# The inverse of the attention's sums moved from VectorE's reciprocal to ScalarE's logarithm and exponential, and the turning of the maxima moved behind key tile 3

## The chip, the cores and the metric

The kernel runs on one core of one Trainium2 chip. The metric is the device time of one execution in microseconds. Three runs of the kernel before took 669.23, 670.58 and 672.26 us; the median is 670.58 us. PE is TensorE, ACT is ScalarE, DVE is VectorE, POOL is GpSimd, SP is SyncE, whose queue issues most DMAs.

## The reference, cut to what matters

Three stages follow each other: attention in which a query sees only the keys of its own hash bucket, a dense layer with a softmax gate and a layer norm (called SoLU here), and a mixture of eight experts with one expert for each token. The change touches only the attention:

```python
mask = q_bucket[:, :, :, None] == k_bucket[:, :, None, :]
scores = scale * np.matmul(q, k.transpose(0, 1, 3, 2))      # 16 heads, 768 x 768, depth 64
scores = np.where(mask, scores, -1000000000.0)
scores = scores - np.max(scores, axis=-1, keepdims=True)
attn = np.exp(scores)
attn = attn / (np.sum(attn, axis=-1, keepdims=True) + 1e-09)
return np.matmul(attn, v).astype(np.float32)
```

The kernel doesn't divide the weights. It multiplies weights by values first, and then scales the 64 x 768 result of a head by the inverse of each query's sum.

## The kernel before, in words

The attention takes the 16 heads one after the other (`for h in range(HEADS)`), each in six key tiles kt of 128 keys. Each engine has its own instruction list, written out by hand in program order, and the lists meet at semaphores. There is no scheduler: an instruction that waits holds everything behind it on its engine.

Head h on each engine:

- PE, for each kt: first two matmuls of a head further on, which produce scores only for finding maxima (`leading`, L472, head h+2 from kt 2 on, absent in heads 14 and 15), then four matmuls for the two query halves (`products`, L492 and L493). After the products of kt 2 come the sums of head h-1 (`sums(h-1)`, L514, which need all five adds of POOL for that head), the second half of its values (`values`, L504), and then `turn_maxima(h+1)` (L479), a transposition that writes bank RB of PSUM, the bank that also holds the sums. After kt 5 comes the first half of head h's values, which waits until DVE has finished head h-1 (`s_fin`). Heads 0, 2, 4, 6, 8 and 10 end with `hashes` for a later pair of heads.
- ACT: exponentials of the scores for each kt in two halves (`weights_of`, L1033); between them `weights_scaled(h)` (L1046) and, right behind kt 2, `weights_high(h)` (L1050), which prepare one piece of the next stage's weights. In odd heads up to 11 two copies of a later pair (`high_parts`, L1042) stand behind kt 0.
- POOL: in odd heads up to 11 `low_parts` (L1237), then `add(h, 1)` (L1248), then `weights_low(h)` (L1253), which waits for `weights_high(h)` of ACT, then the adds of kt 2 to 5 (L1248). Together the five adds form the head's sums over key tiles.
- DVE: maxima of `leading` (`maximum`, L728); for head h-1 `sums_out` (L748, which adds EPS and takes the sums out of PSUM), three reciprocals of 128 columns each (`inverse`, L753) with `maximum(h+2, 1)` between the second and the third, and `attended` (L759 and L763, which scales the head's result and raises `s_fin`); then `place_maxima(h+1)` (L741).

The semaphores that matter below: `s_acc` (adds of POOL done), `s_wh` (high part of a weight piece done), `s_rb` (sums in bank RB), `s_rec` (steps of DVE on the inverse), `s_fin` (head finished), `s_mt` (maxima turned).

Of the kernel before, what the change touches and what calls it, by code (L numbers as in the profile page):

```python
# [39 lines left out]
ACT = mybir.ActivationFunctionType  # L40
# [3 lines left out]
P = 128  # L44
B, H, S, D = 2, 8, 768, 64
NBITS = 6
HEADS = B * H
TILES = S // P
KT = S // P
HALF = S // 2  # L50
# [4 lines left out]
E = 8  # L55
# [11 lines left out]
EPS = 1e-9  # L67
# [21 lines left out]
C_SLOT = C_LOW + E * E  # L89
C_TOK = C_SLOT + SLOTS  # L90
C_ALT = C_TOK + NT
C_ALL = C_ALT + E - 1


def constants():

    c = np.zeros((P, C_ALL), np.float32)
    c[:, C_ID:C_ID + P] = np.eye(P)


    for group in range(4):
        for head in range(2):
            for n, sign in enumerate((1, -1) if group % 2 == 0 else (-1, 1)):
                r = slice(group * GROUP + head * BITS + n * NBITS, group * GROUP + head * BITS + (n + 1) * NBITS)
                c[r, C_THR] = LEAST if sign > 0 else -ABOVE
                c[r, C_TOP] = -BIG if group % 2 == 0 else 1.0
                if group < 2:
                    c[:, C_SIGN:C_SIGN + P][:, r] = sign
    c[:, C_TRI:C_TRI + P] = np.triu(np.ones((P, P)), 1)
    c[:, C_ONE:C_ONE + P] = 1  # L110
    c[:, C_EXP:C_EXP + E] = np.arange(E) - E
    c[:, C_J:C_J + NT] = np.arange(NT) * P


    c[:, C_J] = -1
    c[:, C_LOW:C_LOW + E * E] = np.tril(np.ones((E, E)), -1).reshape(1, -1)
    c[:, C_SLOT:C_SLOT + SLOTS] = np.arange(SLOTS)
    for n in range(NT):
        c[:, C_TOK + n] = (n % B) * S + (n // B) * P + np.arange(P)
    c[:, C_ALT:C_ALT + E - 1] = (-1.0) ** np.arange(E - 1)  # L120
    return c


# [11 lines left out]
def build(nc, qT, kT, vP, proj_d, w_solu, g_ln, w_gates, w1, w2, cst_d, out):  # L135
    with ExitStack() as ctx:
# [8 lines left out]
        cst = sb("cst", [P, C_ALL])  # L145
# [43 lines left out]
        def many(name, word, n, width, dt=F32):  # L189
            return [at(f"{name}{i}", word + i * width, [P, width], dt)[:, :] for i in range(n)], word + n * width  # L190
# [5 lines left out]
        xch, w = many("xch", 0, 2, DM, F32R)  # L196
        xcl, w = many("xcl", w, 2, DM, F32R)
# [8 lines left out]
        A1, w = many("A1", mid, SETS, S, F32R)  # L206
# [11 lines left out]
        PT = PT.rearrange("p (k g q) -> p k g q", k=KT, g=2)  # L218
        w = (w + 7) // 8 * 8
        acc, w = many("acc", w, 2, S)  # L220
        (rec,), w = many("rec", w, 1, HALF)
        stg, w = many("stg", w, 2, DM)
        empty = at("empty", mid - 2 * DM, [P, ROW])

# [37 lines left out]
        ld_w = [sem(f"ld_w{c}") for c in range(2)]  # L262
        s_high, s_low, s_ws, s_wh, s_wl = sem("s_high"), sem("s_low"), sem("s_ws"), sem("s_wh"), sem("s_wl")
        ld_v = [sem(f"ld_v{c}") for c in range(2)]
        (s_hash, s_bits, s_slot, s_nm, s_mm, s_mt, s_mc, s_st, s_exp, s_acc, s_pv, s_rb, s_rec,
         s_fin, s_ones, s_zeros) = [sem(n) for n in ("s_hash", "s_bits", "s_slot", "s_nm", "s_mm", "s_mt", "s_mc",
                                            "s_st", "s_exp", "s_acc", "s_pv", "s_rb", "s_rec", "s_fin", "s_ones", "s_zeros")]


        m_xh = sem("m_xh")  # L270
# [24 lines left out]
        def wait(eng, s, v):  # L295

            if not isinstance(v, int) or v > 0:
                eng.wait_ge(s, v)
# [153 lines left out]
        def _(pe):  # L452
# [22 lines left out]

            def turn_maxima(h):
                pe.wait_ge(s_mm, h + 1)
                wait(pe, s_rec, 6 * (h - 1) - 5)
                m = pe.transpose(PS[0:TILES, RB, 0:P], mm_[:, h % 2 * TILES:(h % 2 + 1) * TILES], ident)  # L479
                m.then_inc(s_mt, 1)  # L480

# [59 lines left out]
            for h in range(HEADS):  # L541
                for kt in range(KT):
                    ahead = (h + 1, kt + TILES - 2) if kt < 2 else (h + 2, kt - 2)
                    if ahead[0] < HEADS:
                        leading(*ahead)
                    products(h, kt)
                    if kt == 2:
                        if h > 0:
                            sums(h - 1)
                            values(h - 1, (3, 4, 5))  # L550
                        if h + 1 < HEADS:
                            turn_maxima(h + 1)
                values(h, (0, 1, 2))
                if h % 2 == 0 and h // 2 + 2 < PAIRS:
                    pe.wait_ge(s_mc, h + 2)
                    hashes(h // 2 + 2, RB)
# [150 lines left out]
        def _(dve):  # L707
# [35 lines left out]
                                  ident[0:TILES, 0:TILES].unsqueeze(2).broadcast_to([TILES, TILES, P]),  # L743
                                  ALU.mult).then_inc(s_mc, 1)

            def sums_out(h):
                dve.wait_ge(s_rb, h + 1)
                dve.tensor_scalar(rec, PS[:, RB, 0:HALF], EPS, None, ALU.add).then_inc(s_rec, 1)  # L748

            def inverse(h, n):  # L750

                dve.wait_ge(s_rec, 6 * h + 1)
                dve.reciprocal(rec[:, n * P:(n + 1) * P], rec[:, n * P:(n + 1) * P]).then_inc(s_rec, 1)  # L753

            def attended(h):

                p, c = h // 2, h % 2
                dve.wait_ge(s_pv, 2 * h + 2)
                dve.tensor_copy(mu[:, c:c + 1], PS[:, PVB, HALF:HALF + 1]).then_inc(s_rec, 1)  # L759
                dve.wait_ge(s_rec, 6 * h + 5)  # L760
                for g in range(2):
                    mine = slice(g * D, (g + 1) * D)
                    m = dve.scalar_tensor_tensor(  # L763
                        out=xT[c * D:(c + 1) * D, p * S + g * HALF:p * S + (g + 1) * HALF], in0=PS[mine, PVB, 0:HALF],
                        scalar=mu[mine, c:c + 1], in1=rec[mine, :], op0=ALU.add, op1=ALU.mult)
                    m.then_inc(s_rec if g == 0 else s_fin, 1)
# [36 lines left out]
            for h in range(HEADS):  # L803
                if h + 1 < HEADS:
                    maximum(h + 1, TILES - 2)
                    maximum(h + 1, TILES - 1)
                    maxima(h + 1)
                if h % 2 == 1 and h // 2 + 2 < PAIRS:
                    hash_bits(h // 2 + 2, RB)
                if h + 2 < HEADS:  # L810
                    maximum(h + 2, 0)
                if h > 0:
                    sums_out(h - 1)
                    inverse(h - 1, 0)
                    inverse(h - 1, 1)
                if h + 2 < HEADS:
                    maximum(h + 2, 1)
                if h > 0:
                    inverse(h - 1, 2)
                    attended(h - 1)  # L820
                if h + 1 < HEADS:
                    place_maxima(h + 1)
                if h + 2 < HEADS:
                    maximum(h + 2, 2)
                    maximum(h + 2, 3)
            sums_out(HEADS - 1)
            for n in range(3):
                inverse(HEADS - 1, n)
            attended(HEADS - 1)
            soft(0, 0, True)  # L830

# [190 lines left out]
        def _(act):  # L1022
            fn = nc.scalar.activation

            act.dma_start(hashw[:, :], proj_d).then_inc(s_cst, 16)
            act.dma_start(cst[:, :], cst_d).then_inc(s_cst, 16)

            def weights_of(h, kt, g):
                act.wait_ge(s_st, 2 * (KT * h + kt) + g + 1)
                if h > 0 and g == 0:  # L1030
                    act.wait_ge(s_pv, 2 * h - 1 if kt < 3 else 2 * h)
                    act.wait_ge(s_acc, (KT - 1) * (h - 1) + max(kt, 1))
                fn(PT[:, kt, g, 0:HALF], PS[:, STB + g, 0:HALF], ACT.Exp, scale=SCALE).then_inc(s_exp, 1)  # L1033

            def high_parts(p):
                act.wait_ge(ld_r[p % 2], 32 * (p // 2) + 32)
                if p > 0:
                    for h in (2 * p - 2, 2 * p - 1):
                        ready_1(act, h)
                        ready_2(act, h)  # L1040
                for r, high in zip(R[p % 2], (Hq, Hk)):
                    fn(high, r, ACT.Copy).then_inc(s_high, 1)  # L1042

            def weights_scaled(m):
                act.wait_ge(ld_w[m % 2], 16 * (m // 2) + 16)
# [2 lines left out]
            def weights_high(m):  # L1048
                act.wait_ge(s_ws, m + 1)
                fn(piece(m, 0), stg[m % 2], ACT.Copy).then_inc(s_wh, 1)  # L1050
# [26 lines left out]
            for h in range(HEADS):  # L1077
                weights_of(h, 0, 0)
                weights_of(h, 0, 1)
                if h % 2 == 1 and h // 2 + 2 < PAIRS:  # L1080
                    high_parts(h // 2 + 2)
                weights_of(h, 1, 0)
                weights_of(h, 1, 1)
                weights_scaled(h)
                weights_of(h, 2, 0)
                weights_of(h, 2, 1)
                if h == HEADS - 1:
                    act.wait_ge(s_rows0, 16 * SLOTS)
                weights_high(h)
                for kt in (3, 4, 5):  # L1090
                    weights_of(h, kt, 0)
                    weights_of(h, kt, 1)
                if h == HEADS - 2:
                    act.wait_ge(s_fin, HEADS // 2)
                    take(0, 0, 0, True)
            soft(0, 0, True)
            act.wait_ge(s_fin, HEADS)
            take(1, 1, 0, True)
# [263 lines left out]
```

## Time and profile before

| what | value |
|---|---|
| median of three runs | 670.58 us |
| the profiled execution | 669.12 us, span 667.0 us |
| mean granted TensorE clock | 0.956 |
| PE busy | 584.1 us (88%) |
| DVE busy | 402.7 us (60%) |
| POOL busy | 268.8 us (40%) |
| ACT busy | 258.7 us (39%) |
| chain that ended last | PE 75%, ACT 5%, issue 5%, DVE 4%, DMA 4%, POOL 3% |
| three reciprocals a head (L753) | 48 instructions, 42.9 us, 927 ns each |

The span is the time from the first to the last instruction in the profile; the execution's own time is 2.1 us longer. The busy shares are averages over three stages. The attention lies in roughly the first 246 us of the span, the SoLU layer ends near 400 us, and the experts take the rest. The change touches the first of these.

### The profile page before, as it was taken

What the parts mean: (1) busy time and instruction counts of PE and PEld (TensorE: products, weight loads), DVE (VectorE), ACT (ScalarE), POOL (GpSimd) and SP (SyncE); (2) the same over time, 40 slices, a digit from 0 to 9 for tenths busy, and PEclk for the clock granted to TensorE, in tenths of its full rate; (3) what the DMA queues carried; (4) which work ended last, traced back from release to release, by engine and by line L of the source; (5) the groups of instructions that cost most, each with busy time, mean ns of one, the idle gap of its engine ahead of it and who ended that gap; (6) DMA issues with size and microseconds to landing.
All of it is one profiled execution on the core that took longest, in us unless ns stands there. A gap on an engine that the chain in (4) does not pass through costs nothing.

```text
span 667.0 us, 9761 instructions
## 1 busy us (share of the span) xinstructions
PE 584.1 (88%) x2886; PEld 437.3 (66%) x2887; DVE 402.7 (60%) x557; ACT 258.7 (39%) x403; POOL 268.8 (40%) x188
## 2 busy tenths in 40 slices
PE   3889999999999979999999996108999999999994
PEld 1566556556566447888888874007887878788773
DVE  3659888888899546556656662724266455556511
ACT  1255454546554522222222243124255364464410
POOL 4378879888887832322332235530000000100101
PEclk9999999999999998999999997558999999999997
DMA  6789578696571011000000003277146645755400
GB/s 188 168 227 242 155 212 213 158 261 171 124 199 29 12 59 68 1 1 0 0 0 0 0 1 126 91 258 259 56 167 209 240 159 179 270 163 180 151 4 30
DMA packets 39266, 83.90 MB, mean 126 GB/s; under 512 B 7485, under 2 KB 10429, under 8 KB 39232
## 3 DMA queue, kind: packets, MB, share of 16 engines
q1 hardware_dynamic: 31376, 71.04, 36.0%
q10 hardware_dynamic: 5616, 6.12, 3.6%
q0 software_dynamic: 2240, 6.31, 2.4%
q8 instruction: 18, 0.29, 0.2%
q14 instruction: 16, 0.13, 0.1%
HBM read 52.09 MB, written 12.35 MB: 97 GB/s over the span
## 4 chain that ended last, share of the span: by engine, by line
PE 75%; ACT 5%; issue 5%; DVE 4%; DMA 4%; POOL 3%; SPq 2%; ACTq 2%; DVEq 0%; POOLq 0%
PE PS L504 9%; PE PS L492 5%; PE PS L662 5%; PE PS L664 4%; PE PS L663 4%; PE PS L472 4%; PE PS L493 4%; PE PS L535 4%; PE PS L643 3%; PE PS L537 3%; PE PS L536 3%; PE PS L644 3%; PE PS L645 3%; PE PS L576 3%; PE PS L578 3%
## 5 line engine op out<-in xcount | busy, mean ns | idle before, releaser
L1033 ACT ACTIVATE at_PT<-PS 128x384 f32<-128x384 f32 x192 | 84.5, 491 | 100.5 <-PE PS L493 99.8
L1248 POOL TENSOR_TENSOR at_acc<-at_acc,at_PT 128x768 f32<-128x768 f32 x64 | 108.0, 1687 | 8.7 <-ACT at_PT L1033 2.8
L958 DVE TENSOR_TENSOR at_W<-at_raw,at_W 128x2048 f32 (+1 forms) x30 | 67.8, 2289 | 70.8 <-ACT at_W L1103 68.2
L728 DVE TENSOR_REDUCE sb_nm<-PS 128x1 f32<-128x768 f32 x96 | 90.2, 955 | 23.1 <-PE PS L472 18.5
L1324 POOL DMA_INDIRECT out<-at_yb,sb_to x16 | 15.8, 986 | 204.9 <-DVE at_yb L970 204.9
L1103 ACT ACTIVATE at_W<-at_raw 128x2048 f32 (+1 forms) x32 | 60.2, 1910 | 60.3 <-issue 34.5
L492 PE MATMUL PS<-at_A,at_B 102*128 102x384 f32 x192 | 75.1, 391 | 7.6 <-ACT at_PT L1033 7.6
L504 PE MATMUL PS<-at_PT,at_V 128*64 128x385 f32 x384 | 68.4, 489 | 2.4 <-ACT at_PT L1033 2.4
L493 PE MATMUL PS<-at_A,at_B 128*128 128x384 f32 x192 | 66.9, 349 | 0.0
L1279 POOL TENSOR_TENSOR at_cn<-at_eb,sb_mv 128x1024 f32<-128x1024 f32 x12 | 22.7, 1896 | 108.0 <-DVE sb_mv L784 108.0
L472 PE MATMUL PS<-at_B,at_A 76*128 76x384 f32 x192 | 57.9, 390 | 6.7 <-DMA at_B<-at_HB 4.7
L662 PE MATMUL PS<-at_W,at_hTh 128*128 x128 | 52.3, 408 | 5.9 <-DVE at_hTl L989 5.6
L492 PEld LDWEIGHTS PS<-at_A,at_B 102*128 102x128 f32 x192 | 37.5, 196 | 26.6 <-ACT at_PT L1033 20.4
L643 PE MATMUL PS<-at_W,at_xsh 128*128 x128 | 52.1, 407 | 3.2 <-DVE at_xsl L962 3.2
L664 PE MATMUL PS<-at_W,at_hTl 128*128 x128 | 50.5, 394 | 0.0
L644 PE MATMUL PS<-at_W,at_xsh 128*128 x128 | 50.5, 394 | 0.0
L645 PE MATMUL PS<-at_W,at_xsl 128*128 x128 | 50.4, 394 | 0.0
L663 PE MATMUL PS<-at_W,at_hTh 128*128 x128 | 50.4, 394 | 0.0
L504 PEld LDWEIGHTS PS<-at_PT,at_V 128*64 128x64 f32 x384 | 28.0, 136 | 34.2 <-issue 25.8
L472 PEld LDWEIGHTS PS<-at_B,at_A 76*128 76x128 f32 x192 | 36.3, 211 | 20.4 <-DVE sb_nm L728 13.2
L535 PE MATMUL PS<-at_wsp,at_xch 128*128 128x512 f32 x96 | 39.9, 415 | 4.6 <-POOL at_xcl L1258 4.6
L753 DVE RECIPROCAL at_rec<-at_rec 128x128 f32<-128x128 f32 x48 | 42.9, 927 | 0.6
(154 smaller groups left out, 1099.5 us busy)
## 6 DMA issues: line engine op xcount, KB each, us to landing
at_raw<-w SPq DMA_DIRECT2D x32, 1024.0 KB, 5.4
at_A<-at_H SPq DMA_DIRECT2D x32, 192.0 KB, 2.7
at_B<-at_H SPq DMA_DIRECT2D x28, 192.0 KB, 3.7
rows_by_expert<-at_empty SPq DMA_DIRECT2D x19, 257.0 KB, 5.3
at_XS<-rows_by_expert ACTq DMA_DIRECT2D x17, 256.0 KB, 2.7
at_stg<-w_solu SPq DMA_DIRECT2D x16, 256.0 KB, 4.1
at_V<-vP SPq DMA_DIRECT2D x16, 192.0 KB, 3.9
at_Re<-qT SPq DMA_DIRECT2D x4, 384.0 KB, 5.0
```

What stands on the lines that cost most here:

```text
L472: m = mm(slot(h, j)[:, g, :], A1[t][0:ROWS1, j * P:(j + 1) * P], B1[t][0:ROWS1, g * HALF:(g + 1) * HALF], start=True, stop=True)
L492: mm(PS[:, STB + g, 0:HALF], B1[t][0:ROWS, at_k], A1[t][0:ROWS, at_g], start=True, stop=False)
L493: mm(PS[:, STB + g, 0:HALF], B2[t][:, at_k], A2[t][:, at_g], start=False, stop=True).then_inc(s_st, 1)
L504: m = mm(PS[g * D:(g + 1) * D, PVB, 0:HALF + 1], V[h % 2][:, kt, :], PT[:, kt, g, :], start=(kt == 0), stop=(kt == KT - 1))
L643: mm(PS[:, g, :], xsh[:, x_k], W[:, high], start=(k == 0), stop=False)
L644: mm(PS[:, g, :], xsh[:, x_k], W[:, low], start=False, stop=False)
L662: mm(PS[:, 4 + c, :], hTh[:, h_f], W[:, high], start=(f == 0), stop=False)
L663: mm(PS[:, 4 + c, :], hTh[:, h_f], W[:, low], start=False, stop=False)
L664: m = mm(PS[:, 4 + c, :], hTl[:, h_f], W[:, high], start=False, stop=(f == FB - 1))
L728: dve.tensor_reduce(nm[:, col:col + 1], slot(h, j), AX.XY, ALU.max, negate=True).then_inc(s_nm, 1)
L1033: fn(PT[:, kt, g, 0:HALF], PS[:, STB + g, 0:HALF], ACT.Exp, scale=SCALE).then_inc(s_exp, 1)
L1248: pool.tensor_tensor(total, PT[:, 0, :, 0:HALF] if kt == 1 else total, PT[:, kt, :, 0:HALF], ALU.add).then_inc(s_acc, 1)
```

## The change

The inverse of a head's sums is computed in another way. ACT takes the logarithm of the sum plus EPS straight out of PSUM into `rec`, and then exp(-x) of it in place. DVE makes one Newton step: the first instruction forms err = (sum + EPS) * rec, the second rec = (2 - err) * rec. The two replace `sums_out` and the three reciprocals. `maximum(h+2, 1)` now stands ahead of both.

On ACT the two new instructions stand behind the exponentials of kt 2, and `weights_high(h)` moves from there to behind those of kt 3. On PE `turn_maxima(h+1)` moves from behind the values of kt 2's block to behind the products of kt 3, and its wait on `s_rec` now names the first Newton instruction of head h-1, which is the last reader of bank RB. An activation table set that holds both functions is loaded by name at the start. The constants grow by one column with EPS in it, and a buffer `err` of 384 columns joins `rec`.

```diff
-        (rec,), w = many("rec", w, 1, HALF)
+        (rec, err), w = many("rec", w, 2, HALF)
...
             def turn_maxima(h):
                 pe.wait_ge(s_mm, h + 1)
-                wait(pe, s_rec, 6 * (h - 1) - 5)
+                wait(pe, s_rec, 4 * (h - 1) - 3)
...
                             values(h - 1, (3, 4, 5))
-                        if h + 1 < HEADS:
-                            turn_maxima(h + 1)
+                    if kt == 3 and h + 1 < HEADS:
+                        turn_maxima(h + 1)
...
-            def sums_out(h):
-                dve.wait_ge(s_rb, h + 1)
-                dve.tensor_scalar(rec, PS[:, RB, 0:HALF], EPS, None, ALU.add).then_inc(s_rec, 1)
-
-            def inverse(h, n):
-
-                dve.wait_ge(s_rec, 6 * h + 1)
-                dve.reciprocal(rec[:, n * P:(n + 1) * P], rec[:, n * P:(n + 1) * P]).then_inc(s_rec, 1)
+            def inverse(h):
+
+                dve.wait_ge(s_ln, 2 * h + 2)
+                dve.scalar_tensor_tensor(out=err, in0=PS[:, RB, 0:HALF], scalar=EPS, in1=rec,
+                                         op0=ALU.add, op1=ALU.mult).then_inc(s_rec, 1)
+                dve.wait_ge(s_rec, 4 * h + 1)
+                dve.scalar_tensor_tensor(out=rec, in0=err, scalar=2.0, in1=rec, reverse0=True,
+                                         op0=ALU.subtract, op1=ALU.mult).then_inc(s_rec, 1)
...
                 if h + 2 < HEADS:
                     maximum(h + 2, 0)
-                if h > 0:
-                    sums_out(h - 1)
-                    inverse(h - 1, 0)
-                    inverse(h - 1, 1)
                 if h + 2 < HEADS:
                     maximum(h + 2, 1)
                 if h > 0:
-                    inverse(h - 1, 2)
+                    inverse(h - 1)
                     attended(h - 1)
...
+            act.preload_act_table_set("natural_log_exp_and_others")
...
+            def inverse(h):
+
+                act.wait_ge(s_rb, h + 1)
+                wait(act, s_fin, h)
+                fn(rec, PS[:, RB, 0:HALF], ACT.Ln, bias=cst[:, C_EPS:C_EPS + 1]).then_inc(s_ln, 1)
+                act.wait_ge(s_ln, 2 * h + 1)
+                fn(rec, rec, ACT.Exp, scale=-1.0).then_inc(s_ln, 1)
...
                 weights_of(h, 2, 0)
                 weights_of(h, 2, 1)
+                if h > 0:
+                    inverse(h - 1)
                 if h == HEADS - 1:
                     act.wait_ge(s_rows0, 16 * SLOTS)
-                weights_high(h)
                 for kt in (3, 4, 5):
                     weights_of(h, kt, 0)
                     weights_of(h, kt, 1)
+                    if kt == 3:
+                        weights_high(h)
```

ACT in head 2, before, from the scaling of the weight piece on. at_stg is the piece, at_wsp its high part, at_PT the exponentials of one half, those of kt 2 in the second and third row.

```order
L1046 ACTIVATE at_stg_85<-at_stg_85,sb_gcol 128x512 [waits ld_w0]
L1033 ACTIVATE at_PT_81<-PS 128x384 [waits s_acc,s_pv,s_st]
L1033 ACTIVATE at_PT_81<-PS 128x384 [waits s_st]
L1050 ACTIVATE at_wsp<-at_stg_85 128x512 [waits s_ws]
L1033 ACTIVATE at_PT_81<-PS 128x384 [waits s_acc,s_pv,s_st]
L1033 ACTIVATE at_PT_81<-PS 128x384 [waits s_st]
```

The same place now. L1045 is the logarithm, L1047 the exponential of its negative, L1055 the high part of the piece.

```order
L1051 ACTIVATE at_stg_86<-at_stg_86,sb_gcol 128x512 [waits ld_w0]
L1030 ACTIVATE at_PT_81<-PS 128x384 [waits s_acc,s_pv,s_st]
L1030 ACTIVATE at_PT_81<-PS 128x384 [waits s_st]
L1045 ACTIVATE at_rec_84<-PS,sb_cst 128x384 [waits s_fin,s_rb]
L1047 ACTIVATE at_rec_84<-at_rec_84 128x384 [waits s_ln]
L1030 ACTIVATE at_PT_81<-PS 128x384 [waits s_acc,s_pv,s_st]
L1030 ACTIVATE at_PT_81<-PS 128x384 [waits s_st]
L1055 ACTIVATE at_wsp<-at_stg_86 128x512 [waits s_ws]
```

The high part has gone behind the two exponentials of kt 3, and two instructions on at_rec stand in its old place. POOL's list is unchanged: its wait on `s_wh` is still between the first and the second add.

PE in head 3, before, from the last values matmuls of head 2 on. sb_mm are the maxima being turned, at_B_64 and at_A_56 belong to the leading matmuls of head 5.

```order
L504 MATMUL PS<-at_PT_81,at_V_79 64x385 x5
L479 MATMUL PS<-sb_cst,sb_mm 6x128 [waits s_rec,s_mm]
L472 MATMUL PS<-at_B_64,at_A_56 128x384 [waits s_nm]
L472 MATMUL PS<-at_B_64,at_A_56 128x384
L492 MATMUL PS<-at_A_58,at_B_66 128x384 [waits s_exp]
L493 MATMUL PS<-at_A_62,at_B_70 128x384
L492 MATMUL PS<-at_A_58,at_B_66 128x384 [waits s_exp]
L493 MATMUL PS<-at_A_62,at_B_70 128x384
L472 MATMUL PS<-at_B_64,at_A_56 128x384 [waits s_nm]
```

The same place now (L481 is the turning).

```order
L506 MATMUL PS<-at_PT_81,at_V_79 64x385 x5
L474 MATMUL PS<-at_B_64,at_A_56 128x384 [waits s_nm]
L474 MATMUL PS<-at_B_64,at_A_56 128x384
L494 MATMUL PS<-at_A_58,at_B_66 128x384 [waits s_exp]
L495 MATMUL PS<-at_A_62,at_B_70 128x384
L494 MATMUL PS<-at_A_58,at_B_66 128x384 [waits s_exp]
L495 MATMUL PS<-at_A_62,at_B_70 128x384
L481 MATMUL PS<-sb_cst,sb_mm 6x128 [waits s_rec,s_mm]
L474 MATMUL PS<-at_B_64,at_A_56 128x384 [waits s_nm]
```

The turning has passed the leading matmuls and products of kt 3 and stands, with its two waits, ahead of the leading matmuls of kt 4.

## Rows read from the trace of the kernel before

**Rows 1.** Windows: stretch, its us, busy us by engine, TensorE clock, DMA share, GB/s.
```profile
20.00:60.00 40.00, 35.03 (x153) 25.01 (x155) 27.37 (x36) 19.20 (x39) 27.38 (x17) 1.00 0.80 204
...
100.00:140.00 40.00, 38.60 (x210) 23.89 (x211) 34.12 (x47) 20.96 (x47) 35.05 (x23) 1.00 0.79 197
250.00:255.00 5.00, 3.98 (x9) 3.15 (x10) 3.84 (x10) 0.00 (x0) 3.79 (x3) 0.50 0.59 239
```

**Rows 2.** Timeline of PE, the sums: start, us, engine, line, operation, count, [idle before].
```profile
112.83 0.87 PE L514 MATMUL PS<-at_acc,sb_cst 128*64 128x384 f32 x4
...
127.11 0.87 PE L514 MATMUL PS<-at_acc,sb_cst 128*64 128x384 f32 x4
...
139.57 0.87 PE L514 MATMUL PS<-at_acc,sb_cst 128*64 128x384 f32 x4
...
217.99 0.87 PE L514 MATMUL PS<-at_acc,sb_cst 128*64 128x384 f32 x4
...
229.50 0.87 PE L514 MATMUL PS<-at_acc,sb_cst 128*64 128x384 f32 x4
...
240.65 0.87 PE L514 MATMUL PS<-at_acc,sb_cst 128*64 128x384 f32 x4
```

**Rows 3.** Timeline of PE inside head 6, around the maxima and the values.
```profile
112.56 0.33 PE L493 MATMUL PS<-at_A,at_B 128*128 128x384 f32 x1
...
115.57 0.27 PE L479 MATMUL PS<-sb_cst,sb_mm 128*6 128x128 f32 x1
115.59 0.60 PE L472 MATMUL PS<-at_B,at_A 76*128 76x384 f32 x2
...
116.74 0.51 PE L472 MATMUL PS<-at_B,at_A 76*128 76x384 f32 x2
...
119.00 0.34 PE L493 MATMUL PS<-at_A,at_B 128*128 128x384 f32 x1
119.52 2.16 PE L504 MATMUL PS<-at_PT,at_V 128*64 128x385 f32 x12 [0.18 <-ACT at_PT L1033]
```

**Rows 4.** Timeline of ACT in head 6, and one row of head 14.
```profile
112.74 0.86 ACT L1033 ACTIVATE at_PT<-PS 128x384 f32<-128x384 f32 x2
113.48 0.64 ACT L1050 ACTIVATE at_wsp<-at_stg 128x512 fp32r<-128x512 f32 x1
116.58 0.87 ACT L1033 ACTIVATE at_PT<-PS 128x384 f32<-128x384 f32 x2 [2.46 <-PE PS L493]
...
221.39 0.87 ACT L1033 ACTIVATE at_PT<-PS 128x384 f32<-128x384 f32 x2 [2.12 <-PE PS L493]
```

**Rows 5.** Timeline of POOL in heads 6 and 7.
```profile
114.20 1.29 POOL L1253 TENSOR_TENSOR at_wsp<-at_stg,at_wsp 128x512 fp32r<-128x512 f32 x1 [0.35 <-ACT at_wsp L1050]
...
130.22 1.31 POOL L1253 TENSOR_TENSOR at_wsp<-at_stg,at_wsp 128x512 fp32r<-128x512 f32 x1
131.46 7.19 POOL L1248 TENSOR_TENSOR at_acc<-at_acc,at_PT 128x768 f32<-128x768 f32 x4
```

**Rows 6.** Timeline of DVE in head 6, and at the end of the attention.
```profile
116.23 0.96 DVE L728 TENSOR_REDUCE sb_nm<-PS 128x1 f32<-128x768 f32 x1
117.11 0.94 DVE L753 RECIPROCAL at_rec<-at_rec 128x128 f32<-128x128 f32 x1
...
118.11 1.26 DVE L763 SCALAR_TENSOR_TENSOR at_xT<-PS,sb_mu,at_rec 64x384 f32<-64x384 f32 x2
...
246.43 1.23 DVE L772 TENSOR_REDUCE sb_nm<-PS 128x1 f32<-128x1024 f32 x1 [0.38 <-PE PS L537]
```

**Rows 7.** Timeline of all engines at the first tiles of the SoLU layer.
```profile
249.49 1.27 POOL L1258 TENSOR_TENSOR at_xcl<-at_xT,at_xch 128x512 fp32r<-128x512 f32 x1 [10.19 <-ACT at_xch L1063]
...
251.02 0.77 PE L535 MATMUL PS<-at_wsp,at_xch 128*128 128x512 f32 x1 [4.62 <-POOL at_xcl L1258]
...
251.98 1.90 POOL L1279 TENSOR_TENSOR at_cn<-at_eb,sb_mv 128x1024 f32<-128x1024 f32 x1 [1.22 <-DVE sb_mv L784]
...
252.13 1.76 DVE L789 TENSOR_TENSOR sb_var_all<-sb_var_all,sb_rs 128x1 f32<-128x1 f32 x1
```

More of the change, by code:

```diff
@@ L91 @@
 C_ALT = C_TOK + NT
-C_ALL = C_ALT + E - 1
+C_EPS = C_ALT + E - 1
+C_ALL = C_EPS + 1
 def constants():
@@ L120, in constants @@
     c[:, C_ALT:C_ALT + E - 1] = (-1.0) ** np.arange(E - 1)
+    c[:, C_EPS] = EPS
     return c
@@ L264, in build @@
         ld_v = [sem(f"ld_v{c}") for c in range(2)]
-        (s_hash, s_bits, s_slot, s_nm, s_mm, s_mt, s_mc, s_st, s_exp, s_acc, s_pv, s_rb, s_rec,
+        (s_hash, s_bits, s_slot, s_nm, s_mm, s_mt, s_mc, s_st, s_exp, s_acc, s_pv, s_rb, s_ln, s_rec,
          s_fin, s_ones, s_zeros) = [sem(n) for n in ("s_hash", "s_bits", "s_slot", "s_nm", "s_mm", "s_mt", "s_mc",
-                                            "s_st", "s_exp", "s_acc", "s_pv", "s_rb", "s_rec", "s_fin", "s_ones", "s_zeros")]
+                                            "s_st", "s_exp", "s_acc", "s_pv", "s_rb", "s_ln", "s_rec", "s_fin", "s_ones", "s_zeros")]
         m_xh = sem("m_xh")
@@ L759, in attended @@
                 dve.tensor_copy(mu[:, c:c + 1], PS[:, PVB, HALF:HALF + 1]).then_inc(s_rec, 1)
-                dve.wait_ge(s_rec, 6 * h + 5)
+                dve.wait_ge(s_rec, 4 * h + 3)
                 for g in range(2):
@@ L825, in _ @@
                     maximum(h + 2, 3)
-            sums_out(HEADS - 1)
-            for n in range(3):
-                inverse(HEADS - 1, n)
+            inverse(HEADS - 1)
             attended(HEADS - 1)
@@ L1095, in _ @@
                     take(0, 0, 0, True)
+            inverse(HEADS - 1)
             soft(0, 0, True)
```

## The prediction

> **What bounds the kernel now.** I read the windows by stage first, then the timelines of PE, ACT, POOL and DVE over one head, and then the waits between them. From 100 to 140 us PE is busy for 38.60 of 40 us at a clock of 1.00, DVE for 34.12, POOL for 35.05, ACT for 20.96 [rows 1]. So PE bounds the attention, and POOL is close behind; ACT has room.
>
> I measure a head by the start of its sums matmuls, S. Between S = 127.11 and 139.57 lie 12.46 us, between 112.83 and 127.11, where hashes and two copies of ACT stand too, 14.28 us; the last two intervals take 229.50 - 217.99 = 11.51 and 240.65 - 229.50 = 11.15 [rows 2]. By the loops there are 15 intervals: eight of the first kind, five of the second (hashes stand in heads 2, 4, 6, 8 and 10), and the last two, where the leading matmuls are gone.
>
> One wait of PE inside a head matters. The values of kt 0 to 2 start 0.52 us after the last product, at 119.00 and 119.52, where the same step ahead of the sums takes 0.27 (112.56 to 112.83) [rows 2, 3]. The profile names ACT with 0.18, but those exponentials were done long before. What ended was DVE's scaling of the previous head, at 118.11 + 1.26 = 119.37 [rows 6], and PE followed 0.15 later. So PE loses 0.25 a head to `s_fin`.
>
> **The change part by part.**
>
> *ACT's new work: nothing.* The sums end at S + 0.87 [rows 2]. ACT sits idle for 2.46 us before the exponentials of kt 3, which start at 116.58 = S + 3.75, and the copy that leaves gives 0.64 more [rows 4]. The two new instructions have 384 columns each; the nearest row is a pair of exponentials of that size in 0.87 us, so about 1.0 with their semaphore. They may take up to 2.8 before kt 3 is late, and DVE asks for them only at S + 4.26 (below). A slower logarithm would have to be three times an exponential to show.
>
> *The moved copy: on the path.* POOL's second instruction on the weight piece waits for it, and the four adds of kt 2 to 5 stand behind that in POOL's list. Without the turning the exponentials of kt 3 start 0.02 sooner (the turning shifts the next matmul by 115.59 - 115.57 [rows 3]), at S + 3.73. The second ACT slot behind a pair is at 113.48 - 112.74 = 0.74 [rows 4], so the copy runs from S + 4.47 to S + 5.11, and POOL starts 0.08 later (114.12 to 114.20 [rows 4, 5]), at S + 5.19. Today it does so at S + 1.37. The rest is fixed: 1.24 to the first add (130.22 to 131.46), 7.19 for four adds [rows 5], and 0.25 from POOL's end to PE (250.76 to 251.02 [rows 7]). The next S is therefore at S + 5.19 + 1.24 + 7.19 + 0.25 = S + 13.87 at the earliest. In odd heads POOL also has `low_parts` ahead of this, two instructions that end well before S + 5.
>
> *DVE's Newton step: reads PSUM late.* It stands behind `maximum(h+2, 1)`, which starts at 116.23 and lets the next instruction start at 117.11 [rows 6], that is S + 4.28, now 4.26. For each step I take 0.6, the nearest row being the scaling, two of 384 columns in 1.26 us; lower bound 0.49, one exponential of that size, upper bound the 0.94 of a reciprocal, of only 128 columns. The first step ends at S + 4.86, the second runs from 4.90 to 5.50.
>
> *The lock.* The second step reads two SBUF operands. At 252.13 a DVE operation on one column with two such operands takes 1.76 us and ends at 253.89; POOL's instruction that started at 251.98 ends at 253.88 [rows 7]. So such a DVE operation and a POOL operation do not run together, and the later one waits. Here DVE comes at S + 4.90 and POOL at S + 5.19: POOL waits until 5.50, and the interval becomes 5.50 + 1.24 + 7.19 + 0.25 = 14.18. The Trainium skill (SBUF — State Buffer, "Who interferes with whom") says that a VectorE instruction with two SBUF inputs contends with a GpSimd instruction that reads SBUF and that whichever issues first blocks the other. By that rule, the trace agrees; without it the interval would be the 13.87.
>
> *The turning behind kt 3: a new wait of PE.* It waits for the first Newton step of head h-1, the last reader of bank RB. PE is ready at 116.74 = S + 3.91 [rows 3], where the leading matmuls of kt 4 start today. The step ends at S + 4.86, with 0.15 to PE that is 5.01, and those matmuls start at 5.03: 1.12 later. Behind it on PE stand kt 4 and 5, the values, and the hashes. The 0.25 at `s_fin` goes: PE comes to the values at 6.43 + 1.12 = S + 7.55, DVE's scaling ends at about 5.58 + 1.26 = 6.84, so PE is last. Net 1.12 - 0.25 = 0.87 where PE sets the interval.
>
> *What leaves.* Three reciprocals and the copy out of PSUM leave DVE, which nothing waits for any longer. At the end of the attention DVE's chain is shorter, but its next reduction at 246.43 was released by PE [rows 6], so nothing is gained.
>
> **The sum.** In the eight plain intervals both waits stand side by side. PE alone would need 12.46 + 0.87 = 13.33, POOL's loop 14.18, so the loop decides: 8 x 1.72 = 13.8. In the five with hashes PE needs 14.28 + 0.87 = 15.15, more than the loop: 5 x 0.87 = 4.35. In heads 14 and 15 the sums go first to DVE, early enough for the turning and for the lock, and the kt 3 exponentials start at 221.39 = S + 3.40 [rows 2, 4], so the loop is 3.40 + 0.74 + 0.64 + 0.08 + 1.24 + 7.19 + 0.25 = 13.54, against 11.51 and 11.15: 2.03 + 2.39 = 4.4. In all 22.5 us. The profiled execution took 669.12, so 691.6; on the median of 670.58, which is 1.5 higher, 693.1.
>
> **The rivals.**
>
> *POOL wins the lock.* The margin is only 0.29 us. If POOL's low part starts first at 5.19, DVE waits until 5.19 + 1.27 = 6.46, the second step ends at 7.06, the adds start there, and the interval is 7.06 + 7.19 + 0.25 = 14.50: 8 x 0.32 = 2.6 more. The scaling would end at 7.06 + 0.15 + 1.26 = 8.47, PE go on at 8.62 instead of 7.55, 5 x 1.07 = 5.3 more where PE decides. That is 701. A Newton step longer than I take, or a DVE that is late by 0.3, does it.
>
> *The adds don't gate.* If POOL is faster on the four adds than in the row, or the sums are hidden by PE's own new wait, only the turning costs: 13 x 0.87 = 11.3, so 682. Against it: four adds took 7.19 in the row I use, and the gap to close is 0.85 us.
>
> *The relief of DVE counts: faster.* Place: `s_fin`. Were the new inverse ready so soon that `attended` ends before PE wants the values, PE would gain up to 0.25 in each of 13 heads, 3.3 us, and come to 667. It decides only if the maximum ahead of the inverse ends before S + 3.9 - 0.8, and if the loop over the weight piece stays under 12.46. Both fail by more than 1 us in the rows.
>
> *The clock falls.* PE would be busy for about 85% of a plain interval. From 20 to 60 us it was busy for 35.03 of 40 and the clock stayed at 1.00; after an idle stretch of 4.62 us it was 0.50 [rows 1, 7]. The new waits are at most 2.4 us. If they did it in only four heads, 12 us of PE work at half speed each would add some 48, so 740.
>
> *The change doesn't do what it says.* If the logarithm and exponential each brought a table load, ACT would need more than the gap it has. The instruction list has no such load in the attention, so I give this nothing of its own.
>
> **How the numbers follow.** Forecast 0.60, POOL first 0.18, adds not gating 0.11, clock 0.04, faster 0.03, something that cancels both waits 0.04. The predicted time is 693. The forecast's own range is 688 to 697, from steps of 0.49 to 0.94 us and the interval of 13.87. For 8 in 10 it must reach over the first rival and to the second: 682 to 701. About 0.5% (3.4 us) is what can be told from no change. Faster than that 0.03, within it 0.04, slower 0.93.
>
> **What would show it.** In the profile after, the sums of neighbouring plain heads should stand 14.2 us apart, with PE idle before the sums and released by POOL's adds, and the pairs with hashes 15.1 apart with no such wait. PE should sit idle for about 1.1 us before the turning, released by the first Newton step. POOL should wait before the weight piece until S + 5.2 or 5.5, and its four adds should take 7.2. ACT should still be idle before kt 3, and no table load should stand in the attention. The two later stages should have their old length. I'm wrong if POOL's low part still starts soon after the kt 2 exponentials, if the turning meets no wait, or if a second DVE step of nearly 2 us shows that POOL got the lock.

## The result, and the profile after

The changed kernel takes 690.9 us (median of four runs, 689.62 to 692.69). The ratio to the kernel before is 1.0307 with a 95% interval of 1.0273 to 1.0341: it is slower, by 20 us. The forecast was 693. The profiled execution took 692.69 us with a span of 690.9. It is the longest of the four, at a mean granted clock of 0.937, where the other three have 0.952 to 0.955; two of them lie at 689.6 and 689.7.

The first reading is the chain that ended last, on the page of the changed kernel, in shares of the span by engine. Before, PE held 75% of it and POOL 3%.

```profile
PE 48%; POOL 23%; issue 12%; ACT 4%; DVE 4%; DMA 4%; ACTq 2%; SPq 2%; DVEq 0%; POOLq 0%
```

POOL now holds 23%. The table of waits of the changed kernel, from 60 to 240 us, says who waited for whom: us in total, times, the longest.

```profile
POOL at_wsp L1262 <- ACT at_wsp L1055: 37.2, 13, 3.8
...
PE PS L481 <- DVE at_rec L751: 10.8, 12, 0.9
...
PE PS L516 <- POOL at_acc L1257: 3.7, 8, 0.5
```

Three waits that were not there, or nearly so: POOL for ACT's copy of the weight piece, PE at the turning (L481) for the first Newton step (L751), and PE at the sums (L516) for POOL's adds. The columns of the timelines below are those of [rows 2]: start, duration, engine, line, operation, count, and idle time before with its releaser. First PE, in head 6 of the changed kernel, which answers to [rows 2, 3].

```profile
120.39 0.33 PE L495 MATMUL PS<-at_A,at_B 128*128 128x384 f32 x1
121.19 0.87 PE L516 MATMUL PS<-at_acc,sb_cst 128*64 128x384 f32 x4 [0.47 <-POOL at_acc L1257]
...
123.92 0.62 PE L474 MATMUL PS<-at_B,at_A 76*128 76x384 f32 x2
...
124.91 0.33 PE L495 MATMUL PS<-at_A,at_B 128*128 128x384 f32 x1
126.15 0.27 PE L481 MATMUL PS<-sb_cst,sb_mm 128*6 128x128 f32 x1 [0.90 <-DVE at_rec L751]
126.17 0.59 PE L474 MATMUL PS<-at_B,at_A 76*128 76x384 f32 x2
...
128.63 2.16 PE L506 MATMUL PS<-at_PT,at_V 128*64 128x385 f32 x12
...
136.22 0.87 PE L516 MATMUL PS<-at_acc,sb_cst 128*64 128x384 f32 x4
```

The sums at 121.19 were held 0.47 us by POOL. The turning at 126.15 was held 0.90 us by DVE, where PE was ready at 125.25. The values at 128.63 carry no wait any more. From 121.19 to 136.22 lie 15.03 us, before 14.28. ACT in the same head, to be held against [rows 4]:

```profile
120.57 0.86 ACT L1030 ACTIVATE at_PT<-PS 128x384 f32<-128x384 f32 x2
122.10 0.58 ACT L1045 ACTIVATE at_rec<-PS,sb_cst 128x384 f32<-128x384 f32 x1 [0.67 <-PE PS L516]
122.71 0.52 ACT L1047 ACTIVATE at_rec<-at_rec 128x384 f32<-128x384 f32 x1
124.94 0.87 ACT L1030 ACTIVATE at_PT<-PS 128x384 f32<-128x384 f32 x2 [1.70 <-PE PS L495]
125.70 0.63 ACT L1055 ACTIVATE at_wsp<-at_stg 128x512 fp32r<-128x512 f32 x1
```

The logarithm takes 0.58 and the exponential 0.52, and 1.70 us of idle time is left ahead of kt 3. The copy (L1055) now starts at 125.70. POOL, against [rows 5]:

```profile
117.62 3.52 POOL L1257 TENSOR_TENSOR at_acc<-at_acc,at_PT 128x768 f32<-128x768 f32 x2
121.09 1.54 POOL L1257 TENSOR_TENSOR at_acc<-at_PT 128x768 f32<-128x768 f32 x1
126.40 1.36 POOL L1262 TENSOR_TENSOR at_wsp<-at_stg,at_wsp 128x512 fp32r<-128x512 f32 x1 [3.77 <-ACT at_wsp L1055]
127.73 7.18 POOL L1257 TENSOR_TENSOR at_acc<-at_acc,at_PT 128x768 f32<-128x768 f32 x4
```

POOL's instruction on the weight piece (L1262) waits until 126.40 = S + 5.21. The adds that PE waits for ended at 117.62 + 3.52 = 121.14, 0.05 ahead of the sums. DVE, against [rows 6]:

```profile
119.67 1.48 DVE L737 SCALAR_TENSOR_TENSOR sb_mm<-sb_nm 128x6 f32<-128x6 f32 x1
121.08 0.94 DVE L730 TENSOR_REDUCE sb_nm<-PS 128x1 f32<-128x768 f32 x1
124.58 0.96 DVE L730 TENSOR_REDUCE sb_nm<-PS 128x1 f32<-128x768 f32 x1 [2.56 <-PE PS L474]
125.45 0.55 DVE L751 SCALAR_TENSOR_TENSOR at_rec<-PS,at_rec 128x384 f32<-128x384 f32 x1
126.03 0.56 DVE L754 SCALAR_TENSOR_TENSOR at_rec<-at_rec,at_rec 128x384 f32<-128x384 f32 x1
126.51 0.15 DVE L761 COPY sb_mu<-PS 128x1 f32<-128x1 f32 x1
126.70 1.27 DVE L765 SCALAR_TENSOR_TENSOR at_xT<-PS,sb_mu,at_rec 64x384 f32<-64x384 f32 x2
```

The first step ends at 126.00 = S + 4.81. Nothing waits for the scaling (126.70). At 119.67 the turning's maxima, an instruction on six columns that took 0.17 in every head before, take 1.48 and end at 121.15, with POOL's add.

All intervals between the sums of neighbouring heads, worked out from the starts of the sums in the timelines (medians, where a column holds several; S is the start of a head's sums):

| kernel | S of head 0 | 0 to 1 | seven plain ones | five with hashes | 13 to 14 | 14 to 15 | S of head 15 |
|---|---|---|---|---|---|---|---|
| before | 46.90 | 12.46 | 12.46 | 14.28 | 11.51 | 11.15 | 240.65 |
| after | 48.52 | 15.08 | 13.76 | 15.03 | 13.32 | 15.08 | 263.47 |
| e1_copy_only | 47.40 | 16.01 | 13.69 | 14.35 | 13.32 | 13.38 | 257.77 |
| e2_copy_back | 48.10 | 14.95 | 13.75 (two of 14.1) | 15.91 | 11.67 | 11.25 | 262.44 |
| e3_inverse_first | 46.92 | 15.25 | 13.69 | 14.35 (one of 16.06) | 13.33 | 14.97 | 259.79 |
| e4_both | 47.74 | 13.79 | 12.21 (two of 12.87) | 14.68 (one of 15.14) | 11.67 | 11.28 | 245.13 |
| e5_step_after_max | 47.66 | 13.65 | 12.23 | 14.01 | 11.63 | 11.31 | 239.95 |
| e6_no_second_step | 47.66 | 14.83 | 13.23 | 15.04 | 11.50 | 11.12 | 252.90 |
| e7_err_in_psum | 48.33 | 13.27 | 12.21 | 14.01 | 11.49 | 11.11 | 239.75 |

For the changed kernel this makes 7 x 1.30 = 9.1 us in plain intervals, 5 x 0.75 = 3.8 with hashes, 2.6 in the first, 1.8 and 3.9 in the last two, and 1.6 before the first sums: 22.8 of the span's 23.9. The other 1.1 us lies behind the attention.

The first interval and the last are longer than their pattern by 1.3 and 1.7 us, and there the clock was lower (from 40 to 60 us a mean granted clock of 0.83, before 1.00). In head 1 of the changed kernel ACT waited 3.50 us for a DMA that fills at_B (0.69 before), PE sat idle for 4.48 us until ACT's exponentials were done (1.68 before), and behind that the four sums matmuls took 1.55 us instead of 0.87 and the twelve values matmuls 2.79 instead of 2.11. PE around the last interval, and two windows of the changed kernel (the columns of [rows 1]):

```profile
248.39 0.87 PE L516 MATMUL PS<-at_acc,sb_cst 128*64 128x384 f32 x4 [1.68 <-POOL at_acc L1257]
249.09 3.80 PE L506 MATMUL PS<-at_PT,at_V 128*64 128x385 f32 x12
```

```profile
245.00:250.00 5.00, 3.12 (x15) 1.51 (x16) 0.00 (x0) 2.91 (x7) 4.86 (x4) 0.92 0.00 0
250.00:255.00 5.00, 4.72 (x18) 1.97 (x14) 2.51 (x5) 1.91 (x5) 1.07 (x2) 0.74 0.00 0
```

The same twelve values matmuls take 2.11 us elsewhere and 3.80 here, after 1.68 us of waiting for POOL; the granted clock of the stretch from 250 to 255 is 0.74, a mixture of its two levels, 1.2 and 2.4 GHz.

### The profile page after: what moved, and what is told of

Its sections match the earlier page's. It is cut to its first block, busy times and chain, and to the rows that moved or that the text cites. A ratio compares the mean times of both kernels' runs of the same rounds, so it can differ in the third digit from the quotient of the medians.

```text
span 690.9 us, 9776 instructions
## 1 busy us (share of the span) xinstructions
PE 587.2 (85%) x2886; PEld 435.0 (63%) x2887; DVE 383.2 (55%) x525; ACT 276.2 (40%) x435; POOL 269.1 (39%) x188
## 4 chain that ended last, share of the span: by engine, by line
PE 48%; POOL 23%; issue 12%; ACT 4%; DVE 4%; DMA 4%; ACTq 2%; SPq 2%; DVEq 0%; POOLq 0%
POOL at_acc L1257 16%; PE PS L664 4%; PE PS L666 4%; PE PS L665 4%; PE PS L645 3%; PE PS L537 3%; PE PS L646 3%; PE PS L647 3%; PE PS L539 3%; PE PS L578 3%; PE PS L538 3%; PE PS L580 3%; PE PS L579 3%; POOL at_wsp L1262 3%; POOL rows_by_expert L1323 2%
## 5 line engine op out<-in xcount | busy, mean ns | idle before, releaser
L494 PE MATMUL PS<-at_A,at_B 102*128 102x384 f32 x192 | 73.1, 381 | 10.4 <-ACT at_PT L1030 10.3
L506 PE MATMUL PS<-at_PT,at_V 128*64 128x385 f32 x384 | 70.7, 504 | 0.0
L1288 POOL TENSOR_TENSOR at_cn<-at_eb,sb_mv 128x1024 f32<-128x1024 f32 x12 | 22.8, 1896 | 108.5 <-DVE sb_mv L786 108.5
L474 PEld LDWEIGHTS PS<-at_B,at_A 76*128 76x128 f32 x192 | 34.3, 205 | 28.2 <-issue 16.4
L578 PE MATMUL PS<-at_wsp,at_lnh 128*128 128x512 f32 x96 | 39.2, 408 | 1.7 <-DVE at_lnl L838 1.7
```

The costliest lines, as they stand in the source:

```text
L474: m = mm(slot(h, j)[:, g, :], A1[t][0:ROWS1, j * P:(j + 1) * P], B1[t][0:ROWS1, g * HALF:(g + 1) * HALF], start=True, stop=True)
L494: mm(PS[:, STB + g, 0:HALF], B1[t][0:ROWS, at_k], A1[t][0:ROWS, at_g], start=True, stop=False)
L506: m = mm(PS[g * D:(g + 1) * D, PVB, 0:HALF + 1], V[h % 2][:, kt, :], PT[:, kt, g, :], start=(kt == 0), stop=(kt == KT - 1))
```

## The experiments

The first four share the kernel before at 670.04 us (13 runs); the last three share 670.92 us (18 runs).

**e1_copy_only.** The kernel before, only the copy moved:

```diff
-                weights_high(h)
                 for kt in (3, 4, 5):
                     weights_of(h, kt, 0)
                     weights_of(h, kt, 1)
+                    if kt == 3:
+                        weights_high(h)
```

> The kernel before with one edit: ScalarE's copy weights_high(h) moved behind the exponentials of kt 3; reciprocals and turning as before. Theory (the loop over the weight piece): plain intervals between sums go from 12.46 to about 13.69 us (the 13.76 measured with the change, less the 0.07 that the lock cost), intervals with hashes stay at 14.28, the last two at 13.3 and 13.3 or more: 8 x 1.23 + 1.8 + 2.2 = 13.8 us slower, 684 to 687. Rival (the turning is what costs, the adds don't gate): intervals unchanged, 671.

Measured: 685.77 us, ratio 1.0230 (1.0192 to 1.0269). POOL in head 6, and PE at the sums ahead of and behind it:

```profile
124.73 1.29 POOL L1254 TENSOR_TENSOR at_wsp<-at_stg,at_wsp 128x512 fp32r<-128x512 f32 x1 [3.78 <-ACT at_wsp L1050]
125.98 7.17 POOL L1249 TENSOR_TENSOR at_acc<-at_acc,at_PT 128x768 f32<-128x768 f32 x4
```

```profile
119.51 0.87 PE L514 MATMUL PS<-at_acc,sb_cst 128*64 128x384 f32 x4 [1.17 <-POOL at_acc L1249]
...
133.86 0.87 PE L514 MATMUL PS<-at_acc,sb_cst 128*64 128x384 f32 x4
```

POOL starts on the piece at 124.73 = S + 5.22 and has its adds done at 133.15. The plain intervals are 13.69, as expected. The intervals with hashes became 14.35, where I expected 14.28. The adds are not the reason, since they end 0.71 ahead of the sums at 133.86, and PE's last product starts as late after S as before (14.00 against 14.01). What ends last is on DVE:

```profile
131.77 1.40 DVE L735 SCALAR_TENSOR_TENSOR sb_mm<-sb_nm 128x6 f32<-128x6 f32 x1
133.09 0.67 DVE L722 TENSOR_SCALAR at_HB<-PS,sb_cst 128x384 fp32r<-128x384 f32 x1
```

In these intervals the sums also wait for the hash bits of a later pair (L722, `s_bits`). The maxima's instruction ahead of them (L735) reads SBUF twice, now stands beside POOL's adds and takes 1.40 us, where it took 0.17 in every head before. So the bits end at 133.76, and the sums follow 0.10 later. This is read from the trace; no run takes it apart. So the moved copy alone, with reciprocals and turning as they were, makes 15.7 of the 20 us.

**e2_copy_back.** The changed kernel with the copy back at its old place:

```diff
+                weights_high(h)
                 if h > 0:
                     inverse(h - 1)
...
-                    if kt == 3:
-                        weights_high(h)
```

> The changed kernel with one edit: weights_high(h) back behind the exponentials of kt 2, ahead of the logarithm; turning behind kt 3 and Newton step stay. Theory A (only the wait of the turning is left, lock without effect): plain intervals 12.46 + 0.77 = 13.2, with hashes 15.03, last two as before: 13 x 0.76 = 10 us slower than before, 681. Theory B (the lock counts here): POOL now adds kt 3 from about S + 4.7 to 6.4 when the second Newton instruction wants to start at S + 4.8, so it waits up to 1.6 us and shows a duration near 2.1, the scaling ends at S + 8.3 and PE waits for it: 13 intervals 1.7 longer, 693, no better than the change. Theory C (loop irrelevant): 691 with intervals of 13.76.

Measured: 690.18 us, ratio 1.0290 (1.0254 to 1.0326). No better than the change, though POOL doesn't wait for the copy any more. DVE, POOL and PE in head 6:

```profile
127.18 1.96 DVE L754 SCALAR_TENSOR_TENSOR at_rec<-at_rec,at_rec 128x384 f32<-128x384 f32 x1
```

```profile
127.03 1.69 POOL L1256 TENSOR_TENSOR at_acc<-at_acc,at_PT 128x768 f32<-128x768 f32 x1 [0.39 <-ACT at_PT L1030]
```

```profile
127.29 0.27 PE L481 MATMUL PS<-sb_cst,sb_mm 128*6 128x128 f32 x1 [0.90 <-DVE at_rec L751]
...
130.66 2.16 PE L506 MATMUL PS<-at_PT,at_V 128*64 128x385 f32 x12 [0.81 <-DVE at_xT L765]
```

The second Newton step takes 1.96 us instead of 0.56. It asks at 127.18, while POOL's add of 127.03 to 128.72 runs; the next DVE instruction starts at 129.06. PE then waits 0.81 at the values for the scaling, on top of 0.90 at the turning. Theory B holds, with 690 where it said 693; over all 16 instructions the second step has a median of 1.86 us.

**e3_inverse_first.** The changed kernel with DVE's inverse ahead of the maximum:

```diff
-                if h + 2 < HEADS:
-                    maximum(h + 2, 1)
                 if h > 0:
                     inverse(h - 1)
+                if h + 2 < HEADS:
+                    maximum(h + 2, 1)
+                if h > 0:
                     attended(h - 1)
```

> The changed kernel with one edit on VectorE: both Newton instructions ahead of maximum(h+2, 1), so that the turning's wait is over before PE comes to it; the copy stays behind kt 3. Theory: the wait of 0.90 us before the turning goes, plain intervals stay at 13.7 (the loop over the weight piece sets them), those with hashes return from 15.03 to 14.0 to 14.3: 5 x 0.75 to 1.0 = 4 to 5 us faster than the change, 685 to 687. Rival (the turning sets all intervals): all 13 shorter by 0.8 to 1.0, 679.

Measured: 688.74 us (686.02 to 690.02), ratio 1.0268 (1.0222 to 1.0313), 2.2 under the change, where 4 to 5 was expected. PE from head 5 to 6:

```profile
108.46 0.27 PE L481 MATMUL PS<-sb_cst,sb_mm 128*6 128x128 f32 x1
...
111.05 2.16 PE L506 MATMUL PS<-at_PT,at_V 128*64 128x385 f32 x12
...
118.25 1.48 PE L516 MATMUL PS<-at_acc,sb_cst 128*64 128x384 f32 x4 [1.34 <-POOL at_acc L1258]
```

The turning at 108.46 waits for nothing. The intervals did as the theory said: 13.69 in the plain ones, 14.35 with hashes, as in e1_copy_only. With the turning's wait gone those with hashes could have been as short as the 14.01 of the last experiments. Again the sums follow the hash bits by 0.10: in the next head the maxima's instruction takes 1.60 us, the bits end at 134.21, the sums start at 134.31. One interval of 16.06 and the last of 14.97 took back 1.7 and 1.6 us. The times of this kernel and of the changed one overlap, so it is the intervals that tell them apart, and not the medians. In the row at 118.25 the sums take 1.48 us instead of 0.87, right behind an idle time of 1.34.

**e4_both.** Both edits together, e2_copy_back and e3_inverse_first.

> The changed kernel with both edits: weights_high(h) back behind kt 2 and both Newton instructions ahead of maximum(h+2, 1). Theory without lock: both waits gone, and VectorE's scaling done earlier, 13 x 0.25 less than before: 667 to 668. Theory with lock: the second Newton instruction starts at about S + 3.0 while POOL adds kt 2 (S + 2.6 to 4.3), waits there for 1.3 us in even heads, and pushes maximum(h+2, 1) and the scaling back: PE waits about 0.5 us more than before at the leading matmuls of kt 5 or the values, 674 to 678.

Measured: 670.97 us, ratio 1.0004 (0.9977 to 1.0031). All that the change cost is gone. The time fits neither theory as stated, 667 to 668 without the lock and 674 to 678 with it: the lock is there, but costs less than I had put on it. Intervals with hashes are 14.68 and those of heads 12 and 13 are 12.87. DVE, POOL and PE in an even head:

```profile
117.65 0.56 DVE L751 SCALAR_TENSOR_TENSOR at_rec<-PS,at_rec 128x384 f32<-128x384 f32 x1 [1.80 <-ACT at_rec L1048]
118.24 1.78 DVE L754 SCALAR_TENSOR_TENSOR at_rec<-at_rec,at_rec 128x384 f32<-128x384 f32 x1
119.94 0.94 DVE L730 TENSOR_REDUCE sb_nm<-PS 128x1 f32<-128x768 f32 x1
```

```profile
117.92 1.69 POOL L1257 TENSOR_TENSOR at_acc<-at_acc,at_PT 128x768 f32<-128x768 f32 x1
```

```profile
120.94 0.61 PE L474 MATMUL PS<-at_B,at_A 76*128 76x384 f32 x2 [0.34 <-DVE sb_nm L730]
```

The second step starts at 118.24, beside POOL's add of 117.92 to 119.61, and takes 1.78. The maximum behind it starts at 119.94, and PE's leading matmuls of kt 5 wait 0.34 for it. In plain intervals up to head 11 the step starts when POOL's add has only about 0.2 us left and takes 0.62 to 0.64, and it is POOL's instruction on the piece behind it that takes 1.61 to 1.64 instead of 1.29. They are 12.21, a quarter of a microsecond under the kernel before.

**e5_step_after_max.** e4_both, with the second Newton step (now in `refined`) behind the maximum:

```diff
                 if h > 0:
                     inverse(h - 1)
                 if h + 2 < HEADS:
                     maximum(h + 2, 1)
                 if h > 0:
+                    refined(h - 1)
                     attended(h - 1)
```

> The kernel of e4_both with one edit on VectorE: the second Newton instruction moved behind maximum(h+2, 1), the first stays ahead of it. The lock is still there, but the instruction now asks for it at about S + 4.25, when POOL's add of kt 2 (S + 2.6 to 4.3 in even heads) is ending and the next starts at S + 4.7. Theory (the lock made e4_both lose): the second instruction takes 0.55 to 0.7 instead of 1.78, intervals with hashes fall from 14.68 to 14.0, heads 12 and 13 from 12.87 to 12.2, plain ones stay at 12.2: 4 to 5 us under e4_both, 666 to 667. Rival (something else holds those heads): they stay at 14.68 and 12.87.

Measured: 668.21 us, ratio 0.9961 (0.9945 to 0.9977): faster than the kernel before, by 0.4%. DVE in head 8:

```profile
143.46 0.96 DVE L730 TENSOR_REDUCE sb_nm<-PS 128x1 f32<-128x768 f32 x1 [0.50 <-PE PS L474]
144.33 0.55 DVE L757 SCALAR_TENSOR_TENSOR at_rec<-at_rec,at_rec 128x384 f32<-128x384 f32 x1
```

The step takes 0.55 to 0.57 in 14 of 16 cases, the intervals are 12.23 and 14.01. In two, which lie in the last two intervals, it meets an add of POOL and takes 1.77. The kernel is 2.8 us under e4_both, where I expected 4 to 5. In the two profiled executions the sums of head 15 come 5.2 us sooner, a little more than expected, but from there to the end e4_both took 424.0 us and this kernel 426.2, as the kernel before did (426.4). So the difference to the expectation lies behind the attention; why it was shorter in e4_both isn't known.

**e6_no_second_step.** e2_copy_back without the second Newton step, a copy of one column in its place. The inverse is that of logarithm and exponential alone.

```diff
-                dve.scalar_tensor_tensor(out=rec, in0=err, scalar=2.0, in1=rec, reverse0=True,
-                                         op0=ALU.subtract, op1=ALU.mult).then_inc(s_rec, 1)
+                dve.tensor_copy(err[:, 0:1], err[:, 0:1]).then_inc(s_rec, 1)
```

> The kernel of e2_copy_back without the second Newton instruction: a copy of one column in its place, so the inverse is that of logarithm and exponential alone. The copy has one SBUF input. Theory (the second instruction waited for POOL's add in e2_copy_back, 1.62 to 1.96 us, and PE for it 0.81 us at the values): that wait goes, only the turning's 0.90 stays, plain intervals 13.2, with hashes 15.0: 10 us over before, 680 to 681. Rival (the hold came from elsewhere): intervals stay at 13.75 and 15.9, 690.

Measured: 679.73 us, ratio 1.0137 (1.0111 to 1.0163), 10.5 under e2_copy_back. PE in an even head:

```profile
124.00 0.27 PE L481 MATMUL PS<-sb_cst,sb_mm 128*6 128x128 f32 x1 [0.90 <-DVE at_rec L751]
...
126.49 2.16 PE L506 MATMUL PS<-at_PT,at_V 128*64 128x385 f32 x12
```

The wait of 0.90 at the turning is there, the one at the values is not; the intervals are 13.23 and 15.04. This kernel has the turning's wait by itself, and it costs 0.76 to 0.77 in each of the twelve intervals between heads 1 and 13.

**e7_err_in_psum.** e4_both, with the first step's result in PSUM, over the sums, instead of in SBUF:

```diff
-        (rec, err), w = many("rec", w, 2, HALF)
+        (rec,), w = many("rec", w, 1, HALF)
...
+        err = PS[:, RB, 0:HALF]
...
-                wait(pe, s_rec, 4 * (h - 1) - 3)
+                wait(pe, s_rec, 4 * (h - 1) - 2)
```

> The kernel of e4_both with one edit: the first Newton instruction writes its result over the sums in PSUM bank RB instead of into an SBUF buffer, so that the second has one SBUF and one PSUM input; the turning now waits for the second, which ends at about S + 3.6, before PE comes to it at S + 3.9. Same arithmetic, same order. Theory (two SBUF inputs are what locks): no instruction of 1.78 us any more, intervals 12.2, 14.0 and 12.2, 666 to 667, and POOL's low part falls back from 1.61 to 1.29. Rival (POOL and VectorE disturb each other whatever the operands): as e4_both, 671 with intervals of 14.68 and 12.87.

Measured: 667.88 us, ratio 0.9948 (0.9928 to 0.9968), the lowest median here, though not to be told from e5_step_after_max. The second step's 16 instructions (shortest, median, longest in ns, first and last start), and POOL in head 7:

```profile
L755 DVE SCALAR_TENSOR_TENSOR at_rec<-PS,at_rec x16: 557/557/558, 51.7 to 242.4; 128x384 f32<-128x384 f32 x16
```

```profile
131.17 1.30 POOL L1263 TENSOR_TENSOR at_wsp<-at_stg,at_wsp 128x512 fp32r<-128x512 f32 x1
132.43 7.20 POOL L1258 TENSOR_TENSOR at_acc<-at_acc,at_PT 128x768 f32<-128x768 f32 x4
```

With one operand in PSUM the same arithmetic at the same place (S + 2.95, in e4_both S + 2.94) takes 0.56 in all 16 cases, 15 of which lie beside an instruction of POOL; in e4_both the median was 1.77. POOL's instruction on the piece takes 1.30, where it took 1.61 in the same head there. The intervals are 12.21 and 14.01. So it is the two SBUF operands that lock here, and not that DVE and POOL work side by side. The Trainium skill (SBUF — State Buffer, "Who interferes with whom") states this for two SBUF inputs against a GpSimd instruction that reads SBUF; both sides of it are shown by this pair of runs.

## Why the prediction was right

The forecast was 693 with a range of 682 to 701, and the measured 690.9 came by the mechanism named. That the sum of 22.5 us comes so close to the 22.8 of the profile is luck in part. Plain intervals and those with hashes cost 3.5 us less than the sum had (seven times 1.72 against 9.1, and 4.35 against 3.8). The start, the first interval and the last two cost 3.8 more (1.6 against nothing, 2.6 against 1.7, 5.7 against 4.4), most of it where the clock was lower.

- *PE bounds, POOL close behind.* Right: an edit on ACT alone, which left PE's work untouched, cost 15.7 us (e1_copy_only).
- *ACT's new work costs nothing.* Right. The logarithm takes 0.58 and the exponential 0.52, a little over the 0.49 of the row; 1.70 us of idle time is left before kt 3.
- *The moved copy sets plain intervals.* Right in mechanism; I said 14.18, it was 13.76. The start of POOL's instruction was S + 5.19 by the sum and S + 5.21 in the trace. Two terms were too large. The way from POOL's end to PE took 0.05 and not the 0.25 of [rows 7], where PE waited for another instruction of POOL. And the lock cost about 0.07, the difference between 13.76 and the 13.69 of e1_copy_only, not 0.31: POOL is recorded as starting at 126.40, while DVE's step began at 126.03, and the next DVE instruction already starts at 126.51, so the step seems to have held POOL until about 126.5 and not for its full recorded time.
- *The Newton step's place, and the turning's wait.* Right: 0.87 by the sum, 0.75 measured in intervals with hashes. The step ended at S + 4.81 instead of S + 4.86, and PE had no wait at the values, as forecast. e6_no_second_step shows this wait alone, e3_inverse_first removes it.
- *Heads 14 and 15.* 2.03 and 2.39 by the sum. The first was 1.81; the second was 3.93, of which about 1.7 is the lower clock. There the step "the new waits are at most 2.4 us" stood against a fall of the clock, and it fell behind a wait of 1.68 us. In e1_copy_only the values behind the same wait (1.67 us) took 2.11 us, so it falls in some executions and not in others.
- *The first heads.* The sum took S of head 0 as unchanged and the first interval as plain. S of head 0 came 1.6 us later, and the first interval was 1.3 us longer than the plain ones. It is longer than them in every kernel here but the one before, 13.3 to 16.0 us. The one of e7_err_in_psum, whose plain intervals have none of the new waits, is too (13.27 against 12.21): there ACT waited 3.87 us for the same DMA, PE 4.85 us, and the sums took 1.55. So a part of this is the wait for the DMA and the lower clock behind it and not the new waits. Why the DMA comes later is open, and one profile each can't settle it.
- *The rivals.* "POOL wins the lock" didn't happen in the changed kernel, whose second step took 0.56 in all 16 cases, but it did in e2_copy_back and in e4_both, where other edits moved POOL's adds onto the step. "The adds don't gate" is ruled out by e1_copy_only. "The relief of DVE counts" is false for the change, and true once both waits are gone: plain intervals of 12.21 to 12.23 instead of 12.46, which is the 0.25 at `s_fin` that the prediction named. No table load stands in the attention: the three loads of the changed kernel start at 1.7, 434.5 and 439.5 us, and there were three before.

The two costs don't add. In plain intervals the loop over the weight piece hides the turning's wait: e3_inverse_first, which removes that wait and the lock on the piece, changes them by 0.07 alone. Undoing the copy alone gains nothing either, because the lock appears behind it. Only both together give the time back, and only with the lock out of the way do they give more than that.

## What to carry to other kernels

An instruction that moves off a busy engine's way can be the input of another engine's in-order list: look up who waits for it and what stands behind that wait, and add the whole round up to the next instruction of the bounding engine. Where an instruction with a wait is moved past others, compare the time at which its engine now comes to it with the time at which its releaser ends; the later place can be the worse one. And where DVE and POOL work side by side, as here, give a DVE instruction at most one SBUF operand, or place it where POOL is between two instructions.

## What the runs showed of the hardware that was not expected

- The lock takes even tiny instructions: the maxima's instruction on 128 x 6 elements has a median of 1.40 us in the changed kernel and 0.17 before, only because POOL's adds moved onto it. In the changed kernel it cost nothing visible, since DVE was idle for 2.56 us behind it. In e1_copy_only and e3_inverse_first it held back the hash bits, and the sums with them, by 0.07 and about 0.3 us in each interval with hashes.
- A wait of PE of 1.34 to 1.68 us ahead of the sums was followed by a stretch at the lower clock in some executions (1.48 us for four sums matmuls in e3_inverse_first, 3.80 for twelve values matmuls in the changed kernel). Other waits of this length or longer were followed by no fall: seven of the eight of 1.33 to 1.35 us in e3_inverse_first, and the one of 2.07 us in the changed kernel at 263.47, left the sums their 0.87 us. What decides between the cases is open.
- PE follows POOL's last add by 0.05 us in the changed kernel and in all plain intervals of e1_copy_only and e3_inverse_first, where I had taken 0.25 from another pair.
